# Attention in 24 units on one core: the products of q with the state directly behind the scores

## The reference

```python
f = 1.0 / (1.0 + np.exp(-f_logit))          # 4 batches, 8 heads, 768 steps, 48 wide
state = np.zeros((B, H, D, D))
for t in range(S):
    state = f[:, :, t, :, None] * state + np.einsum('bhd,bhe->bhde', k[:, :, t], v[:, :, t])
    y[:, :, t] = np.einsum('bhd,bhde->bhe', q[:, :, t], state)
```

## Time and profile before

| | |
|---|---|
| median of 3 runs | 822.5 us (822.42 to 822.59) |
| the profiled execution | 822.51 us |
| its span, first to last instruction | 820.7 us |
| mean granted clock of TensorE | 0.994 of full |
| attention, scores of unit 0 to the last `turn_y` | 13.02 to 164.13 us |
| one unit in the middle, scores to scores | 97.67 to 104.18 us |
| routing, last `turn_y` to the first expert matmul | 164.13 to 204.35 us |
| experts, to the end | 204.35 to 820.7 us |

### The profile page before, as it was taken

How to read it: one execution, slowest core, us unless ns; L and a number is a source line. 1 busy time by engine, 2 the same in 40 slices (tenths; PEclk the granted TensorE clock), 3 DMA queues, 4 the chain that set the end, 5 groups by cost and what they waited for, 6 DMA issues and landing times.

```text
span 820.7 us, 15030 instructions
## 1 busy us (share of the span) xinstructions
PE 796.5 (97%) x5785; PEld 762.9 (93%) x5785; DVE 355.8 (43%) x653; ACT 317.8 (39%) x626; POOL 329.4 (40%) x247
## 2 busy tenths in 40 slices
PE   7999999985999999999999999999999999999996
PEld 6888888844999999999999999999999999999996
DVE  7888888555243314323332333243224323331432
ACT  4666777612143314323332333143223323331332
POOL 3678888956144116322602440153216024401001
PEclk9999999998999999999999999999999999999999
DMA  9999999643112012210221030122102210200000
GB/s 152 175 202 193 190 197 190 156 165 107 31 55 100 30 30 78 78 58 0 77 77 58 11 142 10 48 77 77 54 3 77 77 58 0 77 0 30 1 1 29
DMA packets 126801, 64.97 MB, mean 79 GB/s; under 512 B 102448, under 2 KB 119856, under 8 KB 126768
## 3 DMA queue, kind: packets, MB, share of 16 engines
q1 hardware_dynamic: 123696, 55.09, 30.1%
q0 software_dynamic: 3072, 9.44, 3.6%
HBM read 55.07 MB, written 9.44 MB: 79 GB/s over the span
## 4 chain that ended last, share of the span: by engine, by line
PE 94%; DVE 3%; issue 1%; DMA 1%; POOL 0%; ACT 0%; POOLq 0%; DVEq 0%; ACTq 0%
PE psum L1714 24%; PE psum L1716 24%; PE psum L1715 24%; PE psum L1438 4%; PE psum L1498 3%; PE psum L1525 3%; PE psum L1480 2%; PE psum L1541 2%; PE psum L1534 1%; PE psum L1509 1%; PE psum L1725 1%; PE psum L1433 1%; PE psum L1630 0%; DMA f_in<-in_f_logit_dram 0%; DMA xs<-x_rows,ids 0%
## 5 line engine op out<-in xcount | busy, mean ns | idle before, releaser
L1418 DVE SCALAR_TENSOR_TENSOR psum<-rg,psum 128x384 f32<-128x384 f32 x128 | 72.0, 563 | 153.5 <-ACT rg L987 153.5
L987 ACT ACTIVATE rg<-psum,three 128x384 f32<-128x384 f32 x128 | 74.5, 582 | 151.9 <-PE psum L1716 151.9
L1714 PE MATMUL psum<-yh,w_high 128*128 128x384 f32 x384 | 129.7, 338 | 0.1
L1714 PE MATMUL psum<-w_high,gh 128*128 128x384 f32 x384 | 128.4, 334 | 0.3 <-DVE gl L1421 0.3
L1716 PE MATMUL psum<-yh,w_low 128*128 128x384 f32 x384 | 128.4, 334 | 0.0
L1715 PE MATMUL psum<-yl,w_high 128*128 128x384 f32 x384 | 128.3, 334 | 0.0
L1716 PE MATMUL psum<-w_high,gl 128*128 128x384 f32 x384 | 128.3, 334 | 0.0
L1715 PE MATMUL psum<-w_low,gh 128*128 128x384 f32 x384 | 128.3, 334 | 0.0
L806 POOL DMA_INDIRECT out_dram<-ys,ids x24 | 24.0, 1001 | 247.2 <-ACT ys L1001 242.3
L1405 DVE SCALAR_TENSOR_TENSOR hl<-psum,hh 128x384 fp32r<-128x384 f32 x64 | 35.7, 558 | 164.8 <-ACT hh L974 142.4
L1421 DVE SCALAR_TENSOR_TENSOR gl<-psum,gh 128x384 fp32r<-128x384 f32 x128 | 71.4, 557 | 72.5 <-ACT gh L991 72.5
(11 more groups left out here) (194 smaller groups left out, 1503.4 us busy)
## 6 DMA issues: line engine op xcount, KB each, us to landing
raw<-in_moe_w_dram SPq DMA_DIRECT2D x15, 1536.0 KB, 6.6
f_in<-in_f_logit_dram SPq DMA_DIRECT2D x24, 192.0 KB, 4.9
k_in<-in_k_dram SPq DMA_DIRECT2D x24, 192.0 KB, 5.3
q_in<-in_q_dram SPq DMA_DIRECT2D x24, 192.0 KB, 5.7
v_in<-in_v_dram SPq DMA_DIRECT2D x24, 192.0 KB, 4.6
x_rows<-x_nat SPq DMA_DIRECT2D x24, 192.0 KB, 3.9
raw<-in_moe_w_in_dram SPq DMA_DIRECT2D x12, 256.0 KB, 4.2
raw<-in_moe_w_out_dram SPq DMA_DIRECT2D x12, 256.0 KB, 3.2
```

What stands on the lines that cost most here:

```text
L987: act.activation(rg[:, j % 2, :], banks[j % 3][:, 0:CAP], ACT.Relu, bias=three[:, 0:1]).then_inc(r_done, 1)
L1418: dve.scalar_tensor_tensor(out=bank, in0=rg[:, j % 2, :], scalar=6.0, in1=bank, op0=ALU.min, op1=ALU.mult).then_inc(gg_done, 1)
L1714: pe.matmul(bank, high, rhs_high, start=start, stop=False)
```

## The change

In `unit` of TensorE the state products with their two waits and their signal move from behind `turn_y` to directly behind the scores, ahead of the flag's matmul (unit 23 only), the kn, k and q turns and `turn_y`. Nothing else changes: same instructions, same waits, same buffers.

```diff
@@ -1498,6 +1498,17 @@
                 last.then_inc(a_ready, 1)
+                if start_of(n) >= B:
+                    pe.wait_ge(state_done, n - B + 1)
+                if start_of(n) >= 1:
+                    pe.wait_ge(yT_copied, n)
+                pe.sem_inc(passed, 1)
+                for h in range(H):
+                    g, j = h // 2, h % 2
+                    r = slice(HALF * j, HALF * j + HALF)
+                    last = pe.matmul(yT_ps[r, P * g:P * g + P], state[r, b, g, :], q_sc[r, i, P * g:P * g + P],
+                                     start=(g == 0), stop=False, skip_group_check=True)
+                last.then_inc(y_init, 1)
                 if not more_state(tt) and b == B - 1:
                     pe.wait_ge(steep_rows, 1)
                     pe.wait_ge(exp_done, NT)
@@ -1514,17 +1525,6 @@
                     turn_q(n + 1, tt + (b + 1) // B, (b + 1) % B)
                 if start_of(n) >= 1:
                     turn_y(n - 1, 1 - i)
-                if start_of(n) >= B:
-                    pe.wait_ge(state_done, n - B + 1)
-                if start_of(n) >= 1:
-                    pe.wait_ge(yT_copied, n)
-                pe.sem_inc(passed, 1)
-                for h in range(H):
-                    ...
-                last.then_inc(y_init, 1)
                 pe.wait_ge(loaded_v[b], 16 * (tt + 1))
```

## The result

| | before | after |
|---|---|---|
| median of 6 runs (lowest to highest) | 822.46 us (822.29 to 824.07) | 825.89 us (825.10 to 826.06) |
| ratio | | 1.0036, 95% interval 1.0026 to 1.0046 |
| profiled execution, its span | 822.51, 820.7 us | 825.1, 823.4 us |
| granted clock | 0.994 | 0.991 |

The kernel became 3.4 us slower. The profiled execution of after is its fastest, 0.8 under the median; it has 2.6 to 2.7 us of the 3.4.

What follows compares the result with a forecast made beforehand. TensorE, holding 94% of the chain, was taken as the bound. The terms 0 + 0.6 + 2.7 - 0.2 = +3.1 us on a median of 822.5 gave 825.6 us, range 822.8 to 828.8.

Steps and rivals of the forecast that it cites:

- Part 1: TensorE's moved state products: 1.02 us as before, still five shape changes a unit, so 0.
- Part 2: Work pushed back 1.02 us: POOL and loads stay hidden; just-met yT waits in units 5 to 20 cost +0.6 us.
- Rival 1: The just-met wait costs 0.19 us in each of 16 units, 3.0 instead of 0.6: 828.0 us; chance 0.27.
- rival 4: Something unseen, like POOL's decay running into VectorE's scan, up to 0.5 us a unit, ends above forecast; chance 0.06.
- Part 3: Last three units: yT is late behind ScalarE's three casts, last turn_y +2.7 us, nothing given back.
- Part 4: Opening: state products fill unit 1's wait for kv_sum, unit 2's scores then hang on q_sc: -0.2 us.

Runs made afterwards that it cites:

- e5: The kernel after with one more small ScalarE copy, into a tile nobody reads, ahead of l_part in units 4 to 19: 824.45 us.
- e6: The kernel after with four more small ScalarE copies, into a tile nobody reads, ahead of l_part in units 4 to 19: 828.49 us.
- e1: The kernel after with the old order in units 21 to 23, so the new order in units 0 to 20 only: 823.60 us.
- e2: The kernel before with the new order in units 21 to 23 alone: 824.61 us.
- e8: The kernel before with the new order in units 0 to 3 only: 822.65 us.
- e4: The kernel after with ScalarE's casts of units 20 to 23 moved ahead of its copies out of x_ps: 825.66 us.
- e7: The kernel after with the last unit's f loaded ahead of the chunks and the casts of units 20 to 23 ahead of the x_ps copies: 825.10 us.
- e3: The kernel after with the load of the last unit's f issued ahead of the weight chunks on SyncE: 825.54 us.
- e9: e1 with the load of the last unit's f issued ahead of the weight chunks on SyncE: 823.70 us.
- e10: e9 with POOL's last decay step of units 22 and 23 cut from 512 columns to 64: 868.91 us, on another path behind the attention, not comparable.

## Why the prediction was right, and where its sum was not

The sign, the place and the size of the whole were right: 825.6 forecast, 825.89 measured. That the number is so close is in part luck. For waits on yT the sum had 0.6 + 2.7 = 3.3 us and the trace has 2.1; for the load of f and for q_sc it had nothing, and the trace has 0.9.

- **Part 1, TensorE at 0: right.** The unit kept 6.51 us and five idle places.
- **Part 2, "+0.6" for a wait that is just met: wrong.** It measured 0.05 over 16 units. The chain on ScalarE was worked out correctly (forecast 0.14 and 0.06 of slack, the small one in three or four of 16 units; measured 0.17 and 0.08, the small one in four), but the price of 0.19 came from unit 2's scores, of which I took the slack from two other groups' lengths; a slack that is worked out to 0.07 in an irregular unit isn't a measurement. By e5 and e6, slack down to zero costs the state products nothing. What delays unit 2's scores is open: after has them 0.67 behind the f turns instead of 0.59, with 0.10 to spare for q_sc by the same working. Rival 1 falls with it, also in the form that drew on the Trainium skill (TensorE: Matmul & The Clock Gate, Part 1, on queue depths), by which TensorE's queue pulls weight loads ahead of matmuls in flight: a weight load that could not be pulled ahead of the wait would have had to show in each unit, and no unit of after is longer.
- **Part 2, POOL "1.02 us later too; its result is used one unit later" and loads "issued several units ahead": wrong at the end.** This is the rest of the loss, 0.9 of 3.0 us in after's trace and 1.2 by e1. The loads are several units ahead in the steady state, but the last f stands behind chunks that wait for POOL, and it arrived 0.78 late. And POOL's step landed on VectorE's scan: rival 4, at 0.06, had it as up to 0.5 us a unit against 1 us of room. The scan pays 0.8 and the state's multiply gets 0.7 back; they don't both slow down, but the one that begins second does. The room did absorb it in the middle, as the rival said, and in the last units, which are shorter, there is no such room. I had compared POOL's dependencies, not which VectorE instruction it runs beside.
- **Part 3, "+2.7": near as a sum, with other parts.** From unit 20's scores to the last `turn_y` it is 23.85 us instead of 20.89, +2.96 (in the traces' own times the last `turn_y` is 2.61 later, but after's first scores are 0.32 earlier). Of the 2.96, 2.07 are yT's, so this term was 0.6 too large, and 0.89 are f's and q_sc's. Forecast were stalls of the state products of 0.33, 0.9 and 0.84, and a last `turn_y` that hangs on its copy; measured are 0, 0.36 and 0.71, and 1.02 ahead of that `turn_y`. Unit 21's copy of yT starts at 149.18 (forecast 149.54) and ends at 149.76; with the 0.14 it would still be 0.28 late for products at 150.40 - 0.78, but the wait for f covers that, and the wait for q_sc a part of unit 22's: a wait further ahead gives ScalarE time. By itself (e2) the yT part is 2.2.
- **Part 3, "nothing is given back": right.** 656.6 us from the last `turn_y` to the end before, 656.7 after.
- **Part 4, "-0.2": wrong, 0** (e8; in after's own trace unit 2's scores are 0.09 nearer to the first). Two other bounds stand close behind kv_sum's. In e8 the load of f holds unit 1 back by 0.45 more. In e1 it holds it less (unit 0 takes 6.07), and then unit 2's scores wait 0.32 for q_sc, which VectorE starts late for POOL's decay.

Of the 3.4 us, then, some 2.1 to 2.2 arise at yT in the last three units (e2 shows the place, e4 and e7 that it is ScalarE's casts ahead of the copy), and the other 0.9 to 1.2 come from POOL's work at a worse moment, through the load of f (e3, e9) and through VectorE's scan (e10, for unit 22's scores; for unit 21's it is argued). Taking one of them away uncovers a part of the next, so they can't be added exactly. Open is the gap of 1.1 to 1.6 us in e4 and e7, and with it whether the new order with the casts ahead and the scan cleared would reach the kernel before.

## What to carry to other kernels

- When a step of an in-order engine is moved, check the last units apart from the steady ones: with fewer instructions on the bounding engine in them, slack that covered the move is gone. All but 0.06 us of the 3.02 here fell behind the scores of unit 20, in the last 4 of 24 units.
- A wait is worth what its releaser is late (e5: slack of 0.00 and 0.07 us cost nothing); read the slack off two timelines of the same unit, and don't put a price on nearness. And look whether the wait was there before: of the 0.43 for q_sc only 0.08 was new.
- An engine that is moved in time runs beside other work than before. Compare the mean time of each line on the engines that weren't touched: that the scan grew from 1.23 to 2.03 us was in no chain and no wait until the end.

## What the hardware showed that was not expected

- VectorE's scan and POOL's 128x512 operations take turns, and the one that begins second pays. With POOL's decay begun first, the scan is longer by the overlap less some 0.13 us: 1.49 us at an overlap of 0.40 (before, 151.26), 1.56 at 0.47 (after, 151.73), 1.99 at 0.90 (after, 93.29), 2.17 at 1.08 (after, 99.71), against 1.22 with hardly any; POOL's decay keeps its 1.28. With the scan begun first, it keeps its 1.22 and POOL's split takes 2.24 instead of 1.27 (before, 93.72). VectorE's 128x192 multiply takes 1.23 where POOL's multiply began 0.18 ahead of it, and 0.36 where it began 0.18 ahead of POOL's.
- k_sc, which takes one of its two inputs from PSUM, has no part in this: it keeps its 0.69 us and POOL's split its 1.27 where they overlap (before, 101.44 and 101.25).
- The gap within a group of four matmuls with no releaser, 1.10 and 1.57 us, appeared in the two kernels with the casts moved, e4 and e7, and in no other.
- A start-up can differ by 1.8 us between the traces of kernels that are the same up to there (first scores at 11.54 to 13.32), half of what this change is worth. Reading from a point behind it made differences of 0.3 us legible.
